# A three-part attention and expert kernel: expert pieces spread over other turns, filler products in the prologue, row numbers a step sooner, and an end done by thirds

## The reference

```python
# 1: attention, per batch (4) and head (8), 768 steps, head dimension 48
for t in range(S):
    cur = einsum('bhd,bhe->bhde', u * kt, vt)
    y[:, :, t] = einsum('bhd,bhde->bhe', rt, state + cur)
    state = wt[..., None] * state + einsum('bhd,bhe->bhde', kt, vt)
# 2: x (3072 x 384), a hidden layer of 2048
h = x @ w_in
g = h * tanh(log1p(exp(min(h, 20))))        # h where h > 20
x2 = g @ w_out
# 3: 8 experts; (token, expert) pairs are taken in order of falling logit, a token goes to
#    one expert, an expert takes at most 384 tokens
logits = x2 @ w_gate
out[rows of expert e] = maximum(x2[rows of e] @ w1[e], 0) @ w2[e]      # hidden 1024
```

## Time and profile before

| | |
|---|---|
| median of 3 runs | 864.26 us (863.67 to 865.05) |
| profiled execution | 867.02 us, span 865.3 us |
| mean granted TensorE clock | 0.958 of full |
| TensorE busy | 803.1 us (93%), weight loads 598.1 |
| VectorE busy | 655.6 us (76%) |
| ScalarE busy | 405.0 us (47%) |
| GpSimd busy | 290.6 us (34%) |
| bytes moved | 133.50 MB, mean 154 GB/s |
| median landing of a piece's load, of its store | 6.7 us, 5.4 us |

### The profile page before, as it was taken

The page is one execution under the profiler, slowest core; times in us unless marked ns, Lnnn a source line. Parts: engine busy times, 40 slices in busy tenths (PEclk is TensorE's granted clock), DMA queues, the critical chain, the costliest instruction groups (busy, mean ns, idle before and its releaser), DMA issues.

```text
span 865.3 us, 17159 instructions
## 1 busy us (share of the span) xinstructions
PE 803.1 (93%) x6852; PEld 598.1 (69%) x6852; DVE 655.6 (76%) x1105; ACT 405.0 (47%) x655; POOL 290.6 (34%) x245
## 2 busy tenths in 40 slices
PE   7899899999999999999999999583899999999994
PEld 7789778787878787878787867352455655666662
DVE  7678988898979898979897965668668778777220
ACT  2447557575757575767666677600112211212221
POOL 3313453534343434343433450201112312313311
PEclk9699999999999999999999999896699999999998
DMA  8842236363636364545454425304414334335410
GB/s 315 315 161 77 84 101 252 109 246 119 232 134 230 136 223 144 211 155 207 160 201 153 141 98 188 141 2 170 169 29 175 114 115 175 107 123 202 182 46 28
DMA packets 47792, 133.50 MB, mean 154 GB/s; under 512 B 5345, under 2 KB 19809, under 8 KB 45665
## 3 DMA queue, kind: packets, MB, share of 16 engines
q1 hardware_dynamic: 38880, 93.07, 30.1%
q0 software_dynamic: 5376, 34.61, 10.6%
q10 hardware_dynamic: 3456, 4.72, 1.5%
HBM read 97.78 MB, written 34.60 MB: 153 GB/s over the span
## 4 chain that ended last, share of the span: by engine, by line
PE 54%; DVE 26%; issue 10%; DMA 4%; ACT 3%; POOL 2%; SPq 0%; DVEq 0%; ACTq 0%; POOLq 0%
PE bank L403 52%; DVE inv L880 7%; DVE cum L871 4%; DVE t_sb L957 3%; DMA h_sb<-x_rows,ids 3%; DVE h_sb L950 2%; DVE kdiv L888 2%; DVE stage L976 1%; POOL h_sb L1468 1%; DVE cmp L1165 1%; PE bank L641 1%; PE bank L427 1%; ACT t_sb L694 1%; DVE rdec L895 1%; DVE t_sb L1245 1%
## 5 line engine op out<-in xcount | busy, mean ns | idle before, releaser
L1392 POOL TENSOR_TENSOR g_lo<-t_sb,g_hi 128x512 f16<-128x512 f32 x92 | 122.1, 1346 | 120.9 <-ACT g_hi L694 120.9
L403 PE MATMUL bank<-x_hi,win_hi 128*128 128x256 f16 x576 | 159.7, 277 | 1.7 <-DVE x_lo L943 1.7
L403 PE MATMUL bank<-x_lo,win_hi 128*128 128x256 f16 x576 | 159.5, 277 | 0.0
L403 PE MATMUL bank<-x_hi,win_lo 128*128 128x256 f16 x576 | 159.5, 277 | 0.0
L403 PE MATMUL bank<-wout_hi,g_hi 128*128 128x392 f16 (+1 forms) x416 | 130.0, 319 | 8.7 <-ACT g_hi L694 7.9
L403 PE MATMUL bank<-wout_lo,g_hi 128*128 128x392 f16 (+1 forms) x416 | 130.0, 319 | 0.0
L403 PE MATMUL bank<-wout_hi,g_lo 128*128 128x392 f16 (+1 forms) x416 | 129.7, 318 | 0.0
L1376 POOL TENSOR_TENSOR dv<-v_tok,dot 128x384 f32<-128x384 f32 x24 | 39.6, 1649 | 196.1 <-DVE dot L910 196.1
L694 ACT ACTIVATE g_lo<-bank 128x384 f16<-128x384 f32 x64 | 31.4, 490 | 150.0 <-PE bank L403 127.5
L694 ACT ACTIVATE g_hi<-t_sb 128x512 f16<-128x512 f32 x96 | 57.3, 625 | 90.0 <-DVE t_sb L957 66.0
L957 DVE TENSOR_TENSOR t_sb<-t_sb,h_sb 128x512 f32<-128x512 f32 x96 | 91.4, 980 | 6.8 <-ACT t_sb L694 6.8
(11 more groups left out here) (165 smaller groups left out, 1557.4 us busy)
## 6 DMA issues: line engine op xcount, KB each, us to landing
stage<-in_moe_w SPq DMA_DIRECT2D x32, 768.0 KB, 6.7
w_split<-stage SPq DMA_DIRECT2D x32, 768.0 KB, 5.4
wt<-in_w_turned SPq DMA_DIRECT2D x24, 258.0 KB, 5.0
kt<-in_k_turned SPq DMA_DIRECT2D x24, 256.0 KB, 4.5
rt<-in_r_turned SPq DMA_DIRECT2D x24, 256.0 KB, 5.5
r_tok<-in_r SPq DMA_DIRECT2D x24, 192.0 KB, 6.4
k_tok<-in_k SPq DMA_DIRECT2D x24, 192.0 KB, 7.0
v_tok<-in_v SPq DMA_DIRECT2D x24, 192.0 KB, 4.9
```

Of the source, the lines that this page charges most:

```text
L403: return nc.tensor.matmul(*a, **k)
L1392: G.tensor_tensor(g_lo[:, j * GW:(j + 1) * GW], t_sb[:, j * GW:(j + 1) * GW], g_hi[:, j * GW:(j + 1) * GW], ALU.subtract).then_inc(s["glo" ...
```

## The change

Four edits. (1) `split_turns` gives turns 8, 9 and 10 four pieces each and the last turn two; the fourth slot is 7 (VectorE's half in slot 9), the former slots 9 and 11 are gone, and SP handles third and fourth piece together, ahead of the rows of the next block. (2) In the last turn VectorE subtracts all eight remainders, after its last `gated`; the second table load stands behind the eight `rounded`. (3) TensorE's fillers become 24 products at the start, 12 ahead of `scores(1)` and 5 ahead of turn 0. (4) Row numbers: `one_hot_slot` moves ahead of `filled`, `token_ids` from behind step 2 to ahead of `next_step(r, 1)`, and unit I from behind `maxima(r, 1)` to ahead of it. The last expert's Y5, Y6 and Y7 are made at the place of Y7, one third of the rows after the other, and each third is evicted as it ends.

```diff
-            return range(3 * (i - 2), 3 * (i - 1) if i < NI - 1 else PIECES)
-        SPLIT_SLOTS = (1, 3, 5, 9, 11)
+            begin = [3 * (k - 2) + max(0, k - 8) for k in (i, i + 1)]
+            return range(begin[0], min(begin[1], PIECES))
+        SPLIT_SLOTS = (1, 3, 5, 7)
...
-        PLACES = {("A", 0): ["Y1"], ("B", 0): ["H4"], ("A", 1): ["Y2"], ("B", 1): ["H5", "I"],
+        PLACES = {("A", 0): ["Y1"], ("B", 0): ["H4"], ("A", 1): ["Y2", "I"], ("B", 1): ["H5"],
...
-                pieces_of(i, slice(2, 3))
+                pieces_of(i, slice(2, 4))
...
-                elif j % 2 == 0:
-                    pe.wait_ge(s["glo"], NJ * i + j // 2 + 1)
                 else:
-                    pe.wait_ge(s["glov"], j // 2 + 1)
+                    pe.wait_ge(s["glov"], j + 1)
...
-            warm(state[:, :, :].rearrange("p q d -> p (q d)")[:, 0:P], 27)
+            warm(state[:, :, :].rearrange("p q d -> p (q d)")[:, 0:P], 24)
             scores(0)
             pe.wait_ge(s["setup"], 3)
             warm(ident[:, :], 2)
             keys(0)
             values(0)
+            warm(ident[:, :], 12)
             scores(1)
             turn_x(0)
             keys(1)
             values(1)
             turn_x(1)
+            warm(ident[:, :], 5)
             first_stage(turn, finish)
...
+                elif p == E - 1 and f in (F2T - 3, F2T - 2):
+                    pass
+                elif p == E - 1 and f == F2T - 1:
+                    pe.wait_ge(s["hhi"], F2T * E)
+                    pe.wait_ge(s["hlo"], F2T * E)
+                    for m in range(MT):
+                        for g in range(F2T - 3, F2T):
...
+                            last = mm(yb[m][:, 0:DM], lo_, wh, start=False, stop=g == F2T - 1)
+                        last.then_inc(s["ylast"], 1)
...
-                    nc.scalar.preload_act_table_set("sigmoid_and_others")
+                    if i < NI - 1:
+                        nc.scalar.preload_act_table_set("sigmoid_and_others")
...
                     if slot == SLOTS - 1:
                         rounded(i, NJ - 1)
+                        if i == NI - 1:
+                            nc.scalar.preload_act_table_set("sigmoid_and_others")
...
-                    act.wait_ge(s["m2"], F2T * (p + 1))
+                    if p < E - 1:
+                        act.wait_ge(s["m2"], F2T * (p + 1))
...
                     for m in range(MT):
+                        if p == E - 1:
+                            act.wait_ge(s["ylast"], m + 1)
                         A(y_sb[m][:, :], bank[m][:, 0:DM], scale=S_Y).then_inc(s["y"], 1)
...
-                if i == NI - 1 and slot in (11, 13):
+                if slot == 9:
                     expert_piece(i, slot)
-                if slot == 9:
                     gated(i, 0)
...
-                        for j in range(1, NJ, 2):
-                            odd_remainder(i, j)
+                        for j in range(NJ):
+                            last_remainder(i, j)
...
+                if r >= 1:
+                    one_hot_slot(0)
                 filled(r, 0)
                 low_h(old, 3)
-                if r >= 1:
-                    one_hot_slot(0)
                 next_step(r, 0)
                 if r >= 1:
                     by_third()
+                    one_hot_slot(1)
                 filled(r, 1)
                 low_h(old, 4)
                 if r >= 1:
-                    one_hot_slot(1)
+                    token_ids(r - 1)
                 next_step(r, 1)
                 filled(r, 2)
                 low_h(old, 5)
                 next_step(r, 2)
-                if r >= 1:
-                    token_ids(r - 1)
...
-                    if i < NI - 1 or slot % 2 == 1:
+                    if i < NI - 1:
                         remainder(i, slot - NJ - 1)
```

9 lines of the change are left out of this document (7 added, 2 removed).

## The result

The changed kernel takes 856.7 us (median of 6 runs, 854.2 to 857.9), the kernel before 864.65 in the runs beside it: ratio 0.991, 95% interval 0.989 to 0.993. Forecast was 848.3, with a range from 844.5 to 855.5. The direction was right, the size half of what was forecast, and the time lies outside the range.

A forecast was written before the change was run, and what follows sets the result against it. TensorE was taken to bound the kernel, lengthened by its waits. The terms, 8.3 - 4.2 + 3.2 + 1.4 + 7.3 = 16.0, came off the 864.3 us median to give 848.3 us, range 844.5 to 855.5.

The forecast's parts named there:

- What bounds the kernel, and the places: TensorE bounds the kernel and waits at four places: prologue, last turn, search and end; the change touches all four.
- Last turn, minus 8.3: With fewer pieces in the last turn, the reduction that opens the search starts at 552.9 instead of 561.21: 8.3 us.
- The fourth piece, plus 4.2: Turns 8 to 10: a late load delays x_hi, masks and key transposes, costing 2.2, 1.5 and 0.5 us.
- upper bound of 10: Turns 8 to 10: a fourth load landing 3 us later would cost 10 us instead of 4.2.
- The lower bound of 1.5 us: Turns 8 to 10: a fourth load landing as ScalarE gets there costs 1.5 us for the three turns.
- the third rival: Turns 8 to 10: the fourth load comes 3 us later still, as transfers share saturated engines; 854 us, chance 11%.
- The prologue, minus 7.3: Filler products keep the clock full to the first tile, which starts at 28.9 instead of 34.41; gain 7.3 us.
- The first rival: Prologue: the clock falls once more before the first tile, leaving a gain of 2.6 to 5; 851.6 us, chance 30%.
- The row at 49.0: Profile row where the clock fell while TensorE was busy; weighed against full clock at 66 to 69.
- The search, minus 3.2: Search: earlier row numbers remove waits for experts' rows; 1.9 us in round 1, 1.1 in round 2, 0.2 in the others.
- a rival: Fourth load in time, 845.6 us, chance 13%; it added that the reduction across partitions (1.5 us wait) could start sooner.
- The end, minus 1.4: Output: thirds evicted and issued separately, so the last issue starts at 855.65 and not at 857.03.

The follow-up runs named there:

- e15: Changed kernel with GpSimd's even remainders and the second table load ahead of the halves, as before, in the last turn; 860.0 us, ratio 0.996.
- e16: Changed kernel with three raw and three output buffers, four pieces in turns 10 and 11, and the last turn's second table load ahead of the halves; 843.9 us.
- e6: Changed kernel with three raw and three output buffers for the pieces instead of two and two; 844.4 us, ratio 0.975.
- e7: Changed kernel with three raw and three output buffers, three pieces in each of turns 2 to 10 and five in the last; 848.1 us, ratio 0.981.
- e3: Changed kernel with four raw buffers for the pieces instead of two, and two output buffers; 854.5 us, ratio 0.989.
- e9: Changed kernel with the prologue as before: 27 products at the start, none of the 12 and of the 5; 859.6 us, ratio 0.994.
- e11: Changed kernel with the order of the row numbers in the search as before; 856.4 us, ratio 0.990.
- e13: The kernel before, unchanged, run again for a second profile; 862.2 us, ratio 0.999.
- e12: Changed kernel with the last expert's Y5, Y6 and Y7 at their own places and one eviction behind them all; 857.0 us, ratio 0.990.

## Why the prediction was half right

**What bounds the kernel, and the places: right for what was touched.** At all four places the waits that the change aimed at went or shrank (3.1 to 0.4 us in the prologue, 7.9 to 0 in the last turn, 6.8 to 3.6 between 620 and 850 in the search, with other waits in their place). The list of places was not complete: the search was read from 620 on, and 11.0 of the 14.7 us for which TensorE waited for comparisons lie ahead of that, with the long half clock of round 1.

**Last turn, minus 8.3: right** (8.0). The eight groups of logits run without a wait behind sum 7, and the table load with the copies behind it is what is late next, as worked out. Unforeseen was a cost of that place: 1.1 us in e15, though little of it survives (e16).

**The fourth piece, plus 4.2: wrong, and the step that failed.** The mechanism stood there (the load, x_hi, masks, key transposes), and so did its upper bound of 10, which is what came: 9.9. What failed is the sentence that let the load land 6.1 us after its issue, as the third piece's does, "the nearest there is". It took 7.7 and 8.7 us in turns 8 and 9. A nearer row was there: this very transfer took 8.1 and 6.7 us in the trace of before. With these two in place of 6.1 the forecast's own working puts the landings 2.0 and 0.6 us later. With the 1.6 and 2.6 us by which the loads came late, and 1.2 for the clock behind the stall, it gives 9.6 of the 9.9. (Turn by turn it fits less well: 5.0 and 4.1 for 5.4 and 3.1, and 0.5 for 1.5 in turn 10.) That the DMA engines had nothing to spare (busy share 1.02) fits, but no run took other transfers away to show it. So the third rival was nearly the case, with 1.6 and 2.6 us of lateness for its 3. It had 11%, for the ten waits that I took as a sign that such loads are only just late were all of the third piece. The lower bound of 1.5 us was wrong too, on the other side: with buffers enough the work costs 0.6 (e6 against e7). And there were two waits in a row, not one: behind the load stood the store of two pieces ago (e3), a wait of ScalarE's that the code has and the profile of before didn't show, since it never ended last. I had not listed it. The half clock after the stall (1.2 us in turn 8) was not in the sum either.

**The prologue, minus 7.3: wrong, the second step that failed.** The term rests on a clock that stays full to the first tile. The first rival came true instead: the clock fell again before the first tile in nine of fourteen profiles, and after it in the others. I took the granted clock of one execution for the kernel's; 34.41 us for the first tile was the latest of five. The medians say 3.4 (e9), inside the 2.6 to 5 of that rival. The Trainium skill (TensorE: Matmul & The Clock Gate, "What's actually happening") has the clock lowered after an idle stretch. The trace is against that as the only way: at 41.6 the clock fell with TensorE busy 10.00 of the 10.00 us ahead. The row at 49.0, which I had against it, deserved more than the row at 66.

**The search, minus 3.2: right in size**, 3.1 by e11 and e13, and in part by luck: round 1 gave 2.7 and not 1.9, with 3.4 us less of half clock that nobody reckoned with, and the later rounds 0.5 and not 1.3. The 5.2 of the first pair of profiles has 2.0 of chance in it.

**The opening of the search: left out of the sum.** I had seen VectorE's wait of 1.5 us and named it in a rival only. It was a term: moving GpSimd's four remainders, which I booked at nothing, took them away from ahead of its reduction, worth 1.6. In e15 the reduction came 4.3 us behind amax instead of 3.2, and with the half clock that followed the way to round 1 grew by 4.1.

**The end, minus 1.4: right** (1.1 by e12).

Summed up from the stages and experiments: 9.9 - 8.0 - 3.1 - 1.6 - 1.1 - 3.4 = -7.3, where the medians of the two sets say -7.9 and -9.3.

**The version that beats both** keeps all edits but one: three raw and three output buffers, and four pieces in turns 10 and 11. It takes 845.0 and 842.9 us in two sets, ratio 0.975 (0.973 to 0.978): 20 us off the kernel before instead of 8. The buffers alone, with the pieces where the change had put them (e6), give 844.4, which is no different. The change as it was made bought the last turn's 8 us (7.0 of them by the pieces) with 9.9 in the turns ahead, and it was the buffers that it lacked, not slots.

## What to carry to other kernels

Before work is moved into a full stage, follow its buffers and not its slots: list every wait that the moved instruction has in the code (load landed, old output stored), and reckon each from the stage it moves into, also those that never show because another ends last. Read the landing time of the very transfer that the moved work will wait for; it stands in the trace even where nothing waits for it yet. A spare buffer from a finished stage can be worth more than a better place. And look at the same stage in several executions before a term rests on it: here the prologue alone moved by 5 us from one to the next, more than three of the five terms.

## What was not expected of the hardware

- GpSimd went from an elementwise operation to its reduction across partitions in 6.00 us (before, e15) and 6.06 (e13), with nothing in between. When it had been idle for 33 us ahead, its reduction began 0.5 us after the start of the instruction that it waited for.
- TensorE's clock fell also with TensorE busy throughout (10.00 of the 10.00 us ahead of 41.6, and the same ahead of 65.5), at places that change between executions of the same code; after a stall of 3.5 us it was down in turn 8 of the changed kernel, and after one of 3.3 in turn 9 it was not.
- On one chip of five VectorE stood 2 us or more in five search rounds until a GpSimd gather was issued.
- In turns 8 and 9 a load of 768 KB took 6.2 and 5.9 us for the third piece of a turn and 7.7 and 8.7 for the fourth, issued 5 us later; in turn 10 it was 5.8 for both.
